# A mixture-of-experts kernel: layer one takes its experts alternately from both ends of their order by count

## The chip, the cores and the metric

One Trainium2 chip, one of its cores. The metric is the device time of the kernel in microseconds, the median of several runs; lower is better. Experts, tiles and sets are counted from 0.

## The reference

Linear attention with 64 heads (8 batches of 8 heads, 576 tokens, 64 features a head) gives 4608 rows of 512. Then two mixture-of-experts layers with 8 experts and one expert per row:

```python
def _moe_ref(x, modality_id, w_gate, modality_bias, w1, w2):
    logits = x @ w_gate + modality_bias[modality_id]
    e_idx = np.argmax(logits, axis=1)
    ...
    for e in range(E):
        mask = e_idx == e
        if not mask.any():
            continue
        h = np.maximum(x[mask] @ w1[e], 0.0)
        out[mask] = gate_w[mask, None] * (h @ w2[e])
```

`w1[e]` is 512 by 1024, `w2[e]` 1024 by 512, all in float32: 4 MB for one expert. Layer two is the same without the modality bias and with a second gate, a sigmoid of `x @ w_output_gate`. How many rows each expert gets follows from the inputs. Worked out from the reference with its inputs, layer one has the counts 1, 0, 29, 0, 0, 5, 2258 and 2315 for experts 0 to 7, so five experts are used; layer two uses all eight (753, 557, 485, 156, 387, 455, 214, 1601).

## The kernel before

**Stages.** About 507 us of attention in 32 steps of two heads, in which the rows of x are stored to `x_tokens` in HBM and each row's token number and weight are scattered into the expert's bin (`bins[0]`). Then layer one in tiles of 128 rows, 43 turns of the tile loop of which 40 hold rows, then layer two likewise (`L` 0 and 1). The rows of a tile are gathered from HBM by the numbers in a bin (`ids`, L466, then `gather`, L473, both on the POOL queue, five tiles ahead); the result of layer one is scattered by token to `y_tokens`, that of layer two to `out` (L495).

**A tile.** On PE, turn `t` of the loop is: first product of tile t (L1272 to L1274, 8 groups of 3 matmuls of 512 columns, two halves); in layer one the transposes of the finished rows of tile t-2 for layer two's router (L1339); transposes of the gathered rows of tile t+1 (L1299); second product of tile t-1 (L1284 to L1286, 8 groups of 3); in layer one the router's logits of tile t-2 (L1367); transposes of tile t's hidden rows (L1379). Products are taken in two parts of float32, a rounded high one and the rest: three matmuls in place of one. ACT makes the high parts (`xh` L657, `hh` L674), DVE the low ones (`xl` L1021, `hl` L1047); ACT's L644 and DVE's L1018 take the two halves of the hidden rows with a relu, DVE's L1041 scales the result into `ys`. In layer one, every fourth tile also takes part in a ranking (`choose2`, `rank2`, `locate2`) that places rows in layer two's bins.

**Weights.** An expert's weights are a set: four pieces of 1 MB, two of `w1` (the W1 half), two of `w2` (the W2 half). `raw` holds one set as loaded. `wts` holds two sets, each in a high and a low part; set g lies in place g % 2. A set is split from `raw` into `wts` by ACT (`round_pieces`, L522: the high part) and DVE (`low_pieces`, L693: the low part). Which tile splits which set stands in the table `turn`, which `plan` writes: the split of set g+1 begins in the tile of set g whose index within its set equals `EARLY`, or in the set's last tile if that comes earlier. In turn t, ACT and DVE do the W1 half, in turn t+1 the W2 half. ACT then issues the load of the set after (`load_after`, L294): its W1 half in turn t+1, its W2 half in turn t+2, each once `raw` is free of the split before. After the last split it loads one more set, which nobody uses. A tile's first product waits for the W1 half of its set (`s_low[L][1]`), its second product for the W2 half.

**The order of experts.** `tables` (L863) gives each expert a key and a rank by it. In layer one: first the expert that had most rows after six of eight batches (`pick_first`; set 0 is loaded and split during the attention, set and rows of tiles 0 to 2 are taken ahead of `tables`), then the used ones by rising count, unused ones last. Every use of the order follows `t_rank` (row numbers `rowi`, tiles per set, `second`, `after`). Layer two goes by falling count, expert 0 first. Layer one's tiles per set are so 19, 1, 1, 1 and 18.

**Loads by SP.** `load_second(L)` loads set 1 once `tables` has written `second[L]` (L893). Behind it on SP's queue: the wait for `plan` (L363), then for i in 0 to 3 the wait until all loads of piece i in layer one have landed and been split (L368), and the load of piece i of layer two's set 0; then the wait for tile 44's rows and `load_second(1)`. At the start of layer two ACT rounds that set in L538 (`round_first`) and DVE makes its low part in L701.

**Queues at the start of layer one.** DVE runs `tables(0)` in turn 0, after tile 0's work, and `plan(0)` in turn 1. ACT waits for `plan` at the start of turn 2. POOL waits for `rowi` (written at the end of `tables`), issues the fetches of row numbers of tiles 3, 4 and 5, then the gather of tile 3, the fetch of 6, the gather of 4.

Of the kernel before, what the change touches and what calls it, by code (L numbers as in the profile page):

```python
# [30 lines left out]
XG = 5  # L31
NXO = 3
NY = 3
EARLY = 2
PICK = 6
SOON = 3
G = 4
# [49 lines left out]
def build(nc, q, k, v, w_phi, modality, w_gate1, bias1, w1a, w2a, w_gate2, w_out2, w1b, w2b, const, out):  # L87
    f32, f32r, i32, bf16 = mybir.dt.float32, mybir.dt.float32r, mybir.dt.int32, mybir.dt.bfloat16
    ALU, ACT, AX = mybir.AluOpType, mybir.ActivationFunctionType, mybir.AxisListType
# [6 lines left out]
    with ctx:  # L96
# [13 lines left out]
        def sem(name):  # L110
# [12 lines left out]
        t_v = sb("t_v", [P, 2, E])  # L123
        t_s = sb("t_s", [P, 2, E])
        t_key, t_rank, t_k, t_end, t_a, t_b, t_d = (sb("t_" + n, [P, E]) for n in
                                                    ("key", "rank", "k", "end", "a", "b", "d"))
        t_m = sb("t_m", [P, 2, E, E])
        t_es, t_last = sb("t_es", [P, E]), sb("t_last", [P, 1])
# [5 lines left out]
        ex, nv, r0, t0 = (sb("j_" + n, [P, TILES]) for n in ("ex", "nv", "r0", "t0"))  # L134
# [163 lines left out]
        def _(eng):  # L298
# [36 lines left out]
            second_reg = [ctx.enter_context(eng.register(f"second{L}")) for L in range(2)]  # L335
            def load_second(L):
                eng.wait_ge(s_sets, L + 1)
                eng.load(second_reg[L], second[L][0:1, 0:1])
                e = eng.snap(second_reg[L])
                for i in range(PPS):  # L340
                    eng.wait_ge(s_low[L][i], 1)
                    raw_load(eng, L, e, i, s_raw[L][i])
# [342 lines left out]
        def _(eng):  # L685
# [20 lines left out]
            def step(ins):  # L706

                nonlocal steps
                steps += 1
                ins.then_inc(s_r, 1)  # L710
                eng.wait_ge(s_r, steps)
# [151 lines left out]
            def tables(L):  # L863
# [18 lines left out]
                else:  # L882
                    step(eng.scalar_tensor_tensor(t_key[:, :], t_v[:, 0, :], float(E), c_("prio"), ALU.mult, ALU.add))
                step(eng.tensor_tensor(t_m[:, 0], t_key[:, :].unsqueeze(1).broadcast_to(ee),
                                       t_key[:, :].unsqueeze(2).broadcast_to(ee), ALU.is_gt))
                step(eng.tensor_reduce(t_rank[:, :], t_m[:, 0], AX.X, ALU.add))
                step(eng.tensor_tensor(t_m[:, 0], t_rank[:, :].unsqueeze(1).broadcast_to(ee),
                                       c_("tile")[:, 0:E].unsqueeze(2).broadcast_to(ee), ALU.is_equal))
                eng.tensor_tensor(t_m[:, 1], t_m[:, 0], t_v[:, 1, :].unsqueeze(1).broadcast_to(ee), ALU.mult)
# [27 lines left out]
            def plan(L):  # L917
# [23 lines left out]
                step(eng.tensor_tensor(r0[:, :], c_("tile"), r0[:, :], ALU.subtract))  # L941
                step(eng.tensor_scalar(t0[:, :], nv[:, :], float(P), None, ALU.is_le))
                step(eng.tensor_scalar(nv[:, :], c_("tile"), t_end[:, E - 1:E], None, ALU.is_lt))
                step(eng.scalar_tensor_tensor(t0[:, :], r0[:, :], float(EARLY), t0[:, :], ALU.is_lt, ALU.mult))
                step(eng.scalar_tensor_tensor(t0[:, :], r0[:, :], float(EARLY), t0[:, :], ALU.is_equal, ALU.add))
                step(eng.tensor_tensor(nv[:, :], nv[:, :], t0[:, :], ALU.mult))
                step(eng.tensor_scalar(t0[:, :], ex[:, :], 1.0, None, ALU.add))
                step(eng.scalar_tensor_tensor(t0[:, :], ex[:, :], t_last[:, :], t0[:, :], ALU.is_lt, ALU.mult))
# [452 lines left out]
```

## Time and profile before

| | |
|---|---|
| median of 3 runs | 1662.55 us (1660.87 to 1669.14) |
| profiled execution | 1657.9 us, span 1656.0 us |
| PE busy | 1555.1 us, 94% of the span |
| DVE, ACT, POOL busy | 823.2, 616.1 and 440.3 us |
| attention | to about 507 us |
| layer one | first matmul at 508.6 us |
| layer two | first rows at 1128.7 us |

The profile's page gives each engine's busy time, its groups of instructions by line with the idle time ahead of them, and the DMA issues. The timeline gives single instructions with start and duration, and in brackets the idle time before one and what ended it. Matmuls are pipelined, so their starts say more than their durations: at the full clock 512 columns start every 0.23 us. A table by windows gives the busy time of each engine in a stretch, the granted clock of TensorE (1.00 is full) and what the DMA engines moved.

### The profile page before, as it was taken

The numbers are of one execution on the slowest core, as the hardware profiler recorded it, in microseconds if no ns is written. First come the engines' busy times: TensorE is split into PE (matmuls) and PEld (weight loads), VectorE is DVE, ScalarE is ACT, GpSimd is POOL, SyncE is SP. The second block draws the span as 40 slices with busy tenths as digits, with TensorE's granted clock in tenths as the row PEclk, the third lists the DMA queues.
The fourth block names the chain that finished last, engine by engine and source line by source line (L and its number), as shares of the span: only waits on it lengthen the run. The fifth ranks groups of instructions, "written<-read, shape, count | busy, mean of one in ns | idle before, by whom it ended". The sixth has DMA issues, their size and how long they took to land. (4 is left out here: it accounts for less than half of the span.)

```text
span 1656.0 us, 32380 instructions
## 1 busy us (share of the span) xinstructions
PE 1555.1 (94%) x9755; PEld 1317.7 (80%) x9755; DVE 823.2 (50%) x1553; ACT 616.1 (37%) x1052; POOL 440.3 (27%) x435
## 2 busy tenths in 40 slices
PE   7999999999998999999599999965999999999996
PEld 5888888888887888888478888854888888888875
DVE  3777777777776433234543323356424223344344
ACT  4666666665651322222422222231322112233332
POOL 2122122123373232233032233224222222222211
PEclk9999999999999999999799999977999999999998
DMA  5333333335624411111462111103414111432343
GB/s 125 85 78 86 80 81 78 81 86 137 174 67 142 147 40 40 40 40 34 159 235 87 40 40 39 40 13 134 153 39 145 48 40 36 150 124 105 105 142 110
DMA packets 184196, 149.94 MB, mean 91 GB/s; under 512 B 131403, under 2 KB 150219, under 8 KB 183504
## 3 DMA queue, kind: packets, MB, share of 16 engines
q1 hardware_dynamic: 143040, 54.92, 12.9%
q0 software_dynamic: 19968, 46.40, 8.8%
q10 hardware_dynamic: 21008, 46.24, 7.8%
q8 instruction: 110, 1.80, 0.5%
q14 instruction: 70, 0.57, 0.1%
HBM read 114.32 MB, written 32.66 MB: 89 GB/s over the span
## 5 line engine op out<-in xcount | busy, mean ns | idle before, releaser
L1272 PE MATMUL bank<-wts,xh 128*128 (+1 forms) x640 | 260.1, 406 | 32.4 <-DVE wts L693 21.5
L1284 PE MATMUL bank<-wts,hh 128*128 (+1 forms) x640 | 257.9, 403 | 3.3 <-DVE hl L1047 3.3
L1274 PE MATMUL bank<-wts,xl 128*128 (+1 forms) x640 | 253.4, 396 | 0.0
L1273 PE MATMUL bank<-wts,xh 128*128 (+1 forms) x640 | 253.3, 396 | 0.0
L1286 PE MATMUL bank<-wts,hl 128*128 (+1 forms) x640 | 251.1, 392 | 0.0
L1285 PE MATMUL bank<-wts,hh 128*128 (+1 forms) x640 | 249.9, 391 | 0.0
L674 ACT ACTIVATE hh<-bank 128x512 fp32r<-128x512 f32 x172 | 93.8, 595 | 372.0 <-PE bank L1379 371.8
L1018 DVE TENSOR_SCALAR hid<-bank 128x512 f32<-128x512 f32 x86 | 59.4, 691 | 262.0 <-PE bank L1274 261.8
L1041 DVE TENSOR_SCALAR ys<-bank,pair 128x512 f32<-128x512 f32 x86 | 64.4, 749 | 237.9 <-PE bank L1286 236.2
L1272 PEld LDWEIGHTS bank<-wts,xh 128*128 128x128 f32 x640 | 122.4, 191 | 58.6 <-issue 34.8
L1233 PE MATMUL p_n<-kvs,qp 128*128 128x100 f32 (+1 forms) x1280 | 160.9, 276 | 3.1 <-ACT kvs L564 1.0
L1233 PEld LDWEIGHTS p_n<-kvs,qp 128*128 128x128 f32 (+1 forms) x1280 | 142.3, 180 | 20.5 <-ACT kvs L564 10.4
L495 POOL DMA_INDIRECT y_tokens<-ys,pair x43 | 43.4, 1010 | 384.3 <-DVE ys L1041 364.4
L1274 PEld LDWEIGHTS bank<-wts,xl 128*128 128x128 f32 x640 | 122.1, 191 | 26.2
L495 POOL DMA_INDIRECT out<-ys,pair x43 | 43.8, 1018 | 371.4 <-DVE ys L1041 371.4
L1284 PEld LDWEIGHTS bank<-wts,hh 128*128 128x128 f32 x640 | 120.7, 189 | 26.8 <-issue 4.2
L1286 PEld LDWEIGHTS bank<-wts,hl 128*128 128x128 f32 x640 | 120.5, 188 | 26.6
L1273 PEld LDWEIGHTS bank<-wts,xh 128*128 128x128 f32 x640 | 122.3, 191 | 24.0 <-issue 0.2
L1285 PEld LDWEIGHTS bank<-wts,hh 128*128 128x128 f32 x640 | 120.8, 189 | 23.2
L1047 DVE TENSOR_TENSOR hl<-bank,hh 128x512 fp32r<-128x512 f32 x172 | 110.9, 685 | 51.7 <-ACT hh L674 51.7
L693 DVE TENSOR_TENSOR wts<-raw,wts 128x2048 f32 x44 | 99.0, 2289 | 62.2 <-ACT wts L522 62.2
L644 ACT ACTIVATE hid<-bank 128x512 f32<-128x512 f32 x86 | 51.5, 598 | 200.0 <-PE bank L1274 191.4
(250 smaller groups left out, 2561.6 us busy)
## 6 DMA issues: line engine op xcount, KB each, us to landing
raw<-in_moe_w ACTq DMA_DIRECT2D x44, 1024.0 KB, 7.4
raw<-in_moe_w SPq DMA_DIRECT2D x16, 1024.0 KB, 8.0
qs<-in_q SPq DMA_DIRECT2D x64, 128.0 KB
ks<-in_k SPq DMA_DIRECT2D x64, 128.0 KB
vs<-in_v SPq DMA_DIRECT2D x64, 128.0 KB
x_tokens<-xo SPq DMA_DIRECT2D x32, 256.0 KB, 2.7
wts<-raw POOLq DMA_DIRECT2D x4, 1024.0 KB, 4.6
bins<-pair,idx POOLq DMA_INDIRECT x83, 3.6
```

Source lines behind the costliest of these rows:

```text
L495: eng.indirect_dma_start(y_dram if L == 0 else out, bass.IndirectOffsetOnAxis(ap=pair2[:, n, 0:1], axis=0), ys[n % NY][:, :], None, bounds ...
L674: eng.activation(hh[:, half * 4:half * 4 + 4, :].rearrange("p a n -> p (a n)"), src[:, :], ACT.Copy).then_inc(s_hh, 1)
L693: eng.tensor_tensor(wts[:, bass.ds(g % 2, 1), 1, cols], raw[:, i, :].unsqueeze(1), wts[:, bass.ds(g % 2, 1), 0, cols].bitcast(f32), ALU.su ...
L1041: eng.tensor_scalar(ys[m % NY][:, :], b_y[:, :], pair2[:, m, 1:2].bitcast(f32), None, ALU.mult).then_inc(s_y, 1)
L1047: eng.tensor_tensor(hl[:, part, :].rearrange("p a n -> p (a n)"), src[:, :], hh[:, part, :].rearrange("p a n -> p (a n)").bitcast(f32), AL ...
L1233: last = eng.matmul(p_n[h][0:m, c * NW:(c + 1) * NW], qp[:, g, cols], kvs[:, h, g, :], start=g == 0, stop=g == 1)
L1272: eng.matmul(dst[:, :], xh[:, c, :], wh, start=c == 0, stop=False)
L1273: eng.matmul(dst[:, :], xh[:, c, :], wl, start=False, stop=False)
L1274: last = eng.matmul(dst[:, :], xl[:, c, :], wh, start=False, stop=c == DC - 1)
L1284: eng.matmul(b_y[:, :], hh[:, c, :], wh, start=c == 0, stop=False)
L1285: eng.matmul(b_y[:, :], hh[:, c, :], wl, start=False, stop=False)
L1286: last = eng.matmul(b_y[:, :], hl[:, c, :], wh, start=False, stop=c == FC - 1)
```

## The change

`EARLY` becomes 3 in layer one and stays 2 in layer two: a set of more than three tiles splits the next one in its tile 3. `load_second(0)` waits for the rows of tiles 3 and 4 as well before it issues set 1. `tables(0)` gets seven DVE instructions that turn a rank r of n used experts into max(min(2r - 1, 2n - 2r), 0), and leave it where that minimum is not above 0 (rank 0 and the unused ones).

```diff
-EARLY = 2
+EARLY = (3, 2)
...
             def load_second(L):
                 eng.wait_ge(s_sets, L + 1)
+                if L == 0:
+                    for t in range(SOON, XG):
+                        eng.wait_ge(s_xin[t], 16)
                 eng.load(second_reg[L], second[L][0:1, 0:1])
...
                 step(eng.tensor_reduce(t_rank[:, :], t_m[:, 0], AX.X, ALU.add))
+                if L == 0:
+                    step(eng.tensor_scalar(t_b[:, :], t_v[:, 0, :], 0.0, 2.0, ALU.is_gt, ALU.mult))
+                    step(eng.tensor_reduce(t_last[:, :], t_b[:, :], AX.X, ALU.add))
+                    eng.tensor_scalar(t_a[:, :], t_rank[:, :], 2.0, -1.0, ALU.mult, ALU.add)
+                    step(eng.tensor_scalar(t_b[:, :], t_rank[:, :], -2.0, t_last[:, :], ALU.mult, ALU.add))
+                    step(eng.tensor_tensor(t_a[:, :], t_a[:, :], t_b[:, :], ALU.min))
+                    step(eng.scalar_tensor_tensor(t_b[:, :], t_a[:, :], 0.0, t_rank[:, :], ALU.is_le, ALU.mult))
+                    step(eng.scalar_tensor_tensor(t_rank[:, :], t_a[:, :], 0.0, t_b[:, :], ALU.max, ALU.add))
...
-                step(eng.scalar_tensor_tensor(t0[:, :], r0[:, :], float(EARLY), t0[:, :], ALU.is_lt, ALU.mult))
-                step(eng.scalar_tensor_tensor(t0[:, :], r0[:, :], float(EARLY), t0[:, :], ALU.is_equal, ALU.add))
+                step(eng.scalar_tensor_tensor(t0[:, :], r0[:, :], float(EARLY[L]), t0[:, :], ALU.is_lt, ALU.mult))
+                step(eng.scalar_tensor_tensor(t0[:, :], r0[:, :], float(EARLY[L]), t0[:, :], ALU.is_equal, ALU.add))
```

`step` lets DVE wait for the instruction's end. `SOON` is 3 and `XG` 5, so the added waits are those for tiles 3 and 4.

## Rows read from the trace of the kernel before

**Rows 1.** The page: busy time by engine, and the costliest group of instructions by line

```profile
PE 1555.1 (94%) x9755; PEld 1317.7 (80%) x9755; DVE 823.2 (50%) x1553; ACT 616.1 (37%) x1052; POOL 440.3 (27%) x435
...
L1272 PE MATMUL bank<-wts,xh 128*128 (+1 forms) x640 | 260.1, 406 | 32.4 <-DVE wts L693 21.5
```

**Rows 2.** Timeline (start, us, engine, line): first matmuls of tiles 24 and 39

```profile
861.76 0.48 PE L1272 MATMUL bank<-wts,xh 128*128 x1
...
1066.58 0.50 PE L1272 MATMUL bank<-wts,xh 128*128 x1
```

**Rows 3.** Timeline of PE: first matmuls of tiles 19, 20, 21 and 22

```profile
764.56 0.48 PE L1272 MATMUL bank<-wts,xh 128*128 x1
...
779.85 0.50 PE L1272 MATMUL bank<-wts,xh 128*128 x1 [1.53 <-DVE wts L693]
...
800.72 0.79 PE L1272 MATMUL bank<-wts,xh 128*128 x1 [7.06 <-DVE wts L693]
...
829.27 0.79 PE L1272 MATMUL bank<-wts,xh 128*128 x1 [12.96 <-DVE wts L693]
```

**Rows 4.** Timeline of ACT and its queue in tile 21, and of DVE in tile 20

```profile
809.82 2.74 ACTq L294 DMA_DIRECT2D raw<-in_moe_w  x4
815.54 1.91 ACT L522 ACTIVATE wts<-raw 128x2048 f32 x1 [5.74 <-DMA raw<-in_moe_w]
...
790.99 8.90 DVE L693 TENSOR_TENSOR wts<-raw,wts 128x2048 f32 x4 [3.12 <-ACT wts L522]
...
800.47 1.27 DVE L1047 TENSOR_TENSOR hl<-bank,hh 128x512 fp32r<-128x512 f32 x2
```

**Rows 5.** Windows: length, busy us of five engines, granted clock, DMA share, GB/s

```profile
535.00:540.00 5.00, 2.49 (x11) 2.06 (x11) 3.61 (x15) 1.66 (x4) 2.95 (x3) 0.83 0.50 145
...
840.00:850.00 10.00, 10.00 (x54) 8.51 (x54) 3.92 (x12) 4.07 (x3) 0.00 (x0) 1.00 0.89 342
...
1600.00:1610.00 10.00, 7.21 (x27) 5.69 (x26) 3.66 (x4) 1.54 (x3) 2.00 (x2) 0.83 0.19 54
```

**Rows 6.** Timeline of several engines, start of layer one, tiles 1 to 4

```profile
517.94 0.17 DVE L879 TENSOR_SCALAR t_a<-t_v 128x8 f32<-128x8 f32 x1
...
520.98 3.27 SPq L294 DMA_DIRECT2D raw<-in_moe_w  x4
...
528.24 0.75 DVE L1041 TENSOR_SCALAR ys<-bank,pair 128x512 f32<-128x512 f32 x1 [2.04 <-PE bank L1286]
...
528.83 0.47 PE L1272 MATMUL bank<-wts,xh 128*128 128x512 f32 x1
...
531.24 0.94 POOL L473 DMA_INDIRECT xin<-x_tokens,pair  x1 [2.47 <-DMA pair<-bins,rowi]
...
537.51 0.66 PE L1299 MATMUL bank<-cst,xin 128*128 128x128 f32 x4 [2.51 <-DMA xin<-x_tokens,pair]
...
538.34 0.60 ACT L644 ACTIVATE hid<-bank 128x512 f32<-128x512 f32 x1 [8.58 <-DVEq L957]
...
546.73 0.48 PE L1272 MATMUL bank<-wts,xh 128*128 x1
...
560.31 0.48 PE L1272 MATMUL bank<-wts,xh 128*128 x1
```

**Rows 7.** DMA issues: median us to landing of row gathers; landings of weight pieces (L294)

```profile
xin<-x_tokens,pair POOLq DMA_INDIRECT x43, 3.5
...
DMA to landing us min/median/max: 4.9/7.5/16.1
```

**Rows 8.** Timeline of PE in layer two: a set's first matmul after an idle

```profile
1603.06 0.64 PE L1272 MATMUL bank<-wts,xh 128*128 x1 [2.79 <-issue]
```

**Rows 9.** Timeline, end of layer one and start of layer two, PE and ACT

```profile
1082.63 0.49 PE L1284 MATMUL bank<-wts,hh 128*128 x1 [1.12 <-DVE hl L1047]
...
1112.94 7.29 ACT L538 ACTIVATE wts<-raw 128x2048 fp32r<-128x2048 f32 x4
...
1128.73 1.11 PE L1299 MATMUL bank<-cst,xin 128*128 128x128 f32 x4 [16.15 <-DMA xin<-y_tokens,pair]
```

## The prediction

> **What bounds the kernel now.** I read the page's engine line first: PE is busy for 94% of the span [rows 1]. So time is to be had only where PE stands idle or runs at its lower clock. Where it waits is in the groups by line: L1272, the first matmul of a tile, waited 21.5 us for DVE's L693, the second step of a weight split [rows 1]. The timeline of PE says where those waits lie. Over tiles 24 to 39 of layer one, which nothing disturbs, a tile takes (1066.58 - 861.76) / 15 = 13.65 us from first matmul to first matmul, the ranking in every fourth tile included [rows 2]. That is the fair price of a tile. Tiles 19 and 24 start at 764.56 and 861.76: 97.20 us for five tiles, whose fair price is 68.25, so **28.95 us are lost** [rows 2, 3].
>
> Why there: PE waits for a split ahead of tiles 20, 21 and 22 [rows 3], so tiles 19, 20 and 21 are a set each. That agrees with the router's counts (2315 rows, then 1, 5 and 29, then 2258). A set's 4 MB are issued only when the set before is split and `raw` is free, and three sets in a row want them within a tile each: at 809.82 four pieces are issued, and ACT gets the first at 815.54, having idled 5.74 us for it [rows 4]. After the two long idles PE works at its lower level (1.2 GHz; the other is 2.4): the first matmul lasts 0.79 us there, after the idle of 1.53 it lasts 0.50 [rows 3].
>
> A second, smaller loss is at the start of layer one. The first matmuls of tiles 2 and 3 are 17.90 us apart [rows 6], 4.25 over the fair price. PE idled 2.51 us for tile 3's rows; that gather was issued at 531.24 and used at 537.51, 6.3 us for what takes 3.5 at the median, and before it POOL had idled 2.47 us for the row numbers [rows 6, 7]. From 520.98 on SP's four pieces of set 1 were in flight [rows 6]. The clock was 0.83 from 535 to 540 [rows 5]; the lower clock after the idle is the rest of the 4.25.
>
> **The new order.** With five used experts the seven new instructions map ranks 1, 2, 3, 4 to 1, 3, 4, 2: the tiles per set become 19, 1, 18, 1, 1 instead of 19, 1, 1, 1, 18. The number of tiles, matmuls, gathers and stores does not change, nor do counts and order of layer two. Splits fall on tiles 3, 19, 23 and 38. Set 2 is loaded from tile 4 on and split at 19, set 3 from tile 20 and split at 23, set 4 from tile 24 and split at 38: the shortest of these has three tiles, 41 us, for four pieces whose landing took at most 16.1 us each [rows 7]. No wait on a load is left in the layer.
>
> **Middle.** Of the five intervals after tile 19 only the first keeps a split within a one-tile set, with its weights long there. It can be read as it stands: 764.56 to 779.85 is 15.29, 1.64 over, at the full clock [rows 3]. In tile 20 DVE has only the second half of set 2 (two pieces) ahead of ys; tile 3 is such a tile today and lost nothing, 546.73 to 560.31 being 13.58 [rows 6]. Gain 28.95 - 1.64 = **27.3 us**. At the other end of the range the idle of 1.53 grows a little and the clock falls. After an idle of 2.79 us in layer two [rows 8] it was 0.83 over 1600 to 1610 [rows 5], 0.17 x 10 = 1.7 us lost: 25.6.
>
> **End of layer one.** Two one-tile sets now lie at its end. Tile 38 to 39 costs again 1.64 us. Then the second half of set 4 is split during tile 39, and tile 39's second product waits for DVE. Measured from the first matmul of a tile, DVE's first two low pieces end at 790.99 + 8.90 / 2 - 779.85 = 15.6 us [rows 3, 4], ys and two hl after them take 800.47 + 1.27 - 799.89 = 1.85 [rows 4], together 17.45, while today that product starts at 1082.63 - 1066.58 = 16.05 [rows 2, 9]. That is 1.4 late, and PE idles about 2.5 us before it (today 1.12). Idles of 2.51 and 2.79 us were followed by the lower clock, one of 1.53 was not [rows 3, 5, 6, 8], so I take the lower clock here too, at the 1.7 us of layer two. No row shows such a tile behind a layer's last split, so both ends: 0 if the idle stays short and the product isn't late; 3.1, and another 1.7 if the clock falls ahead of tile 39 as well. Sum at the end: 1.64 + 1.4 + 1.7 = **4.7 us lost** (1.6 to 6.4).
>
> **Loads at the end.** After the last split ACT loads one more set that nobody uses; SP waits for its landing before it loads set 0 of layer two. Today that comes in tiles 22 and 23, now after tile 39's start T. The unused W1 half is issued a little before ACT's split in that tile, about T+7.5, the W2 half in tile 40's turn of ACT, about T+18.5 (estimates, from the 15.6 and 17.45 above). At 342 GB/s, 3.1 us per MB [rows 5], or at the median landing of 7.5 us [rows 7], SP issues layer two's pieces at about T+15 and T+27, and the last has landed by T+37. They are needed when ACT starts L538: 1112.94 - 1066.58 = 46.4 [rows 2, 9], plus 3.1 for the late end: T+49.5. So 12 us of room and a cost of nothing. What covers them is the routing of the last tiles and `tables` of layer two, through which PE already waits 16.15 us for its first rows [rows 9]; without that cover each us over T+49.5 costs one. Behind these waits SP has queued only set 1 of layer two, which waits for tile 44's rows anyway.
>
> **Start.** The wait in `load_second` moves set 1 from 520.98 to the landing of tile 4's rows. The fetches and gathers of tiles 3 and 4 then have the DMA engines to themselves: the gather takes 3.5 us, and POOL's 2.47 idle goes. The seven added DVE instructions on 8 columns are, at 0.17 each [rows 6], 1.2 us, with what lies between two 1.3. They delay rowi and POOL's fetches by that. Tile 3's gather is issued at 531.24 - 2.47 + 1.3 = 530.1 and lands at 533.6. PE, which idled 2.51 before 537.51, is ready at 535.0: no idle, full clock, gain **4.25**. The 1.3 us don't reach tile 1, since DVE idles 2.04 before ys at 528.24 [rows 6] and `plan` starts after that. Next late would be `plan`, whose end releases ACT at 538.34 [rows 6]; tile 2's hid is then needed by its transposes a good us before tile 3's start at 546.73 - 4.25 = 542.5, so it isn't late. Bounds: gain 4.25 or 0, if the rows still come late, and 1.3 of loss if the added DVE time shows.
>
> **Split one tile later.** Set 1 is issued when tile 4's rows are there, two POOL issues and a gather after 530.1, about 536.5; four pieces at 3.1 us make 549. ACT comes to the split of tile 3 some 8 us after its first matmul, 550.5. So it costs nothing; at tile 2, about 13 us earlier, ACT would have waited for the later load. The set itself isn't used before tile 19.
>
> **A rule against it.** In the rows the gather took 6.3 us beside set 1's load, against 3.5 [rows 6, 7]. The Trainium skill (DMA: Bandwidth & Descriptors, Issuing engines are not separate DMA queues) says that DMAs of all issuing engines run on the same 16 DMA engines and interleave. By that rule the 8 MB moved to the end of the layer slow the stores and fetches of routing there, which is rival 2; the sum takes nothing for it.
>
> **The sum.** -4.25 - 27.31 + 4.74 = **-26.8 us**. The profiled execution (span 1656.0, time 1657.9) would become 1631.1. It lies 4.65 below the median of the runs shown, 1662.55; the difference is level, not work, so the forecast for the median is 1662.55 - 26.8 = **1635.7**. Best end: -4.25 - 27.3 + 1.6 = -30.0, 1632.6. Worst: 0 + 1.3 - 25.6 + 6.4 + 2.8 (one slowed gather) = -15.1, 1647.5. The range begins at 1627, since a median at the profiled execution's level would be 1657.9 - 30.0 = 1627.9.
>
> **Rivals.**
> 1. The start gives nothing: the chain of fetch and gather on POOL, 1.3 us later, makes tile 3 late, not the load. For it: the margin is 1.4 us. Against: 6.3 against 3.5. 1635.7 + 4.25 = 1640.0.
> 2. The moved loads slow the last group's scatter, fetch and gather, three links on PE's path at 6.3 - 3.5 = 2.8 each [rows 6, 7]: 1644.1. Against: those links come last in the wait of 16.15 us before 1128.73 [rows 9], after the last landing at T+37, on today's axis about 1105.
> 3. The clock stays at 2.4 GHz at the end and tile 39's product isn't late: 1632.6.
> 4. The change doesn't do what it says: the three short sets stay together, or `turn` falls on other tiles. The start alone gives 4.25: 1658.3. Against: the map above, worked out for five used experts.
> 5. **Slower:** set 0 of layer two lands late. Its pieces and the unused ones, eight, go one behind another from T+7.5, the last needed by T+55 (ACT rounds one in 1.91 us [rows 4]). It decides from 5.9 us per MB; at the slowest landing, 16.1 each [rows 7], the last lands at T+136: 81 late, 1717. Slower by 0.5% it is from over 10 us per MB. Against: 3.1 us per MB in 840 to 850 [rows 5].
>
> **Chances.** Forecast 0.62 (own range 1631 to 1640), rival 1 0.12, rival 2 0.10, rival 3 0.08, rival 4 0.05, rival 5 0.03. About 0.5%, 8.3 us, is what a measurement of this kernel can tell from no change: below 1654.2 lie the forecast and rivals 1 to 3, 0.92; within, rival 4, 0.05; slower, rival 5, 0.03. The range 1627 to 1648 takes in all but rivals 4 and 5.
>
> **What will show it.** Start: SP's four pieces of set 1 at about 536, no idle of L1299 for xin, tiles 2 and 3 some 13.6 apart. Middle: one idle of 1.5 us ahead of tile 20, none of ACT for a DMA, tiles 19 to 24 in about 70 us. End: an idle of 1.5 before tile 39, one of about 2.5 before its second product, ACT's L538 without a wait for a DMA, PE's wait for the first rows of layer two still about 16 us. The prediction is wrong if a load is waited for anywhere in layer one, or if the stretch from tile 39's start to layer two's first matmul grows by more than 5 us.

## The result and the profile after

| | before | after |
|---|---|---|
| median of the runs | 1661.71 us (4 runs, 1657.37 to 1669.14) | 1636.91 us (4 runs, 1636.19 to 1640.24) |
| ratio, with its 95% interval | | 0.985 (0.9812 to 0.9889) |
| profiled execution: time, span | 1657.9, 1656.0 us | 1636.26, 1634.4 us |
| first matmul of tile 0 | 508.64 | 511.85 |
| tile 2 to 3 | 17.90 | 13.54 |
| tile 19 to 24 | 97.20 | 69.62 |
| tile 38 to 39 | 13.99 | 16.73 |
| tile 39 to the first matmul of layer two | 68.41 | 72.55 |

The change saves 24.8 us between the medians; 26.8 had been forecast, and 1635.7 for the time. The last five lines of the table are start times and intervals of first matmuls (x-times-W1) in the two timelines of PE. Their differences are +3.21, -4.36, -27.58, +2.74 and +4.14 us. With +0.26 us in the interval from tile 36 to 37 they make -21.6 us, the whole difference of the spans, so nothing else moved by more than hundredths. Layer two takes 12.29 us a tile in both kernels, and 15.34 and 13.88 us for the two tiles at its last split.

The page of after, the engine line of PE and the group that answers to L1272 [rows 1] (busy, mean ns of one | idle before them, and what ended most of it):

```profile
PE 1553.4 (95%) x9755; PEld 1317.6 (81%) x9755; DVE 824.0 (50%) x1560; ACT 616.8 (38%) x1052; POOL 439.6 (27%) x435
...
L1283 PE MATMUL bank<-wts,xh 128*128 (+1 forms) x640 | 258.3, 404 | 15.0 <-DVE xl L1032 8.0
```

The 21.5 us of waiting for the weight split are no longer the largest part of that group's idle time. What is largest now is the 8.0 us behind xl.

The start of layer one, timeline of five engines (start, us, engine, line; in brackets the idle time before it and what ended it), answering to [rows 6]:

```profile
529.82 0.98 POOL L469 DMA_INDIRECT pair<-bins,rowi  x1 [7.01 <-DVE rowi L926]
...
533.63 0.95 POOL L476 DMA_INDIRECT xin<-x_tokens,pair  x1 [0.30 <-issue]
...
538.07 0.60 PE L1310 MATMUL bank<-cst,xin 128*128 128x128 f32 x4
...
540.16 2.21 SPq L294 DMA_DIRECT2D raw<-in_moe_w  x4
...
545.60 0.48 PE L1283 MATMUL bank<-wts,xh 128*128 x1
...
553.17 3.72 ACT L525 ACTIVATE wts<-raw 128x2048 f32 x2 [0.27 <-issue]
...
559.18 0.48 PE L1283 MATMUL bank<-wts,xh 128*128 x1
```

POOL's idle of 2.47 us before the gather is 0.30, PE's transposes of tile 3's rows (L1310) have no idle before them (2.51 us in before), and ACT comes to the split in tile 3's turn (L525) without a wait for a DMA. The set's four pieces (SPq) leave after both gathers.

The middle, timelines of PE, ACT and DVE in tile 19, answering to [rows 3, 4]:

```profile
763.42 0.48 PE L1283 MATMUL bank<-wts,xh 128*128 x1
...
771.12 3.72 ACT L525 ACTIVATE wts<-raw 128x2048 f32 x2 [0.42 <-issue]
...
773.42 4.49 DVE L696 TENSOR_TENSOR wts<-raw,wts 128x2048 f32 x2 [2.00 <-ACT wts L525]
...
778.60 0.50 PE L1283 MATMUL bank<-wts,xh 128*128 x1 [1.42 <-DVE wts L696]
```

One wait of 1.42 us is left of the three of 1.53, 7.06 and 12.96, and it is for the split, not for a load. The four intervals after it are 13.58, 13.58, 13.76 and 13.52 us.

The end of layer one, timelines of PE, ACT, DVE and SP's queue, answering to [rows 9]:

```profile
1024.12 0.50 PE L1283 MATMUL bank<-wts,xh 128*128 x1
...
1032.03 3.72 ACT L525 ACTIVATE wts<-raw 128x2048 f32 x2 [0.42 <-issue]
...
1033.75 0.18 DVE L1015 RECIPROCAL pair<-r_sum 128x4 f32<-128x4 f32 x1
1034.92 4.49 DVE L696 TENSOR_TENSOR wts<-raw,wts 128x2048 f32 x2 [0.99 <-ACT wts L525]
...
1040.85 0.50 PE L1283 MATMUL bank<-wts,xh 128*128 x1 [2.71 <-issue]
...
1057.18 3.86 SPq L294 DMA_DIRECT2D raw<-in_moe_w  x2
...
1057.26 1.12 PE L1350 MATMUL bank<-cst,ys 128*128 128x128 f32 x4 [2.60 <-DVE ys L1052]
1059.12 0.79 PE L1295 MATMUL bank<-wts,hh 128*128 x1
...
1091.36 5.49 ACT L541 ACTIVATE wts<-raw 128x2048 fp32r<-128x2048 f32 x3
...
1107.19 1.12 PE L1310 MATMUL bank<-cst,xin 128*128 128x128 f32 x4 [16.22 <-DMA xin<-y_tokens,pair]
```

Here lie both new losses; RECIPROCAL (L1015) is the last instruction of DVE's position step, which stands ahead of the low pieces in this turn. Tile 39 waits 2.71 us, and its second product (L1295) comes 1059.12 - 1040.85 = 18.27 us after its first matmul, against 16.05 before. Layer two's rounding (L541, three of its four pieces in this view) has no wait for a DMA, and PE waits 16.22 us for layer two's first rows, 16.15 before.

The windows of after around it (length, busy us of PE, PEld, DVE, ACT and POOL, granted clock, DMA share, GB/s):

```profile
1040.00:1050.00 10.00, 9.15 (x44) 7.70 (x45) 2.73 (x6) 1.97 (x4) 5.99 (x6) 1.00 0.38 51
1050.00:1060.00 10.00, 7.40 (x39) 6.27 (x39) 7.14 (x8) 6.21 (x7) 0.98 (x1) 0.82 0.79 247
1060.00:1070.00 10.00, 9.51 (x47) 7.71 (x46) 2.63 (x6) 1.92 (x4) 0.98 (x1) 0.84 1.04 384
```

After the idle of 2.71 us the clock stayed at its upper level; after the one of 2.60 us it fell. The moved loads ran at 384 GB/s while PE had its own work.

### The profile page after: what moved, and what is told of

Same layout as the page of the kernel before. It is cut to its first block and busy times, and to the rows that moved or that the text cites. A ratio compares the mean times of both kernels' runs of the same rounds, so it can differ in the third digit from the quotient of the medians.

```text
span 1634.4 us, 32388 instructions
## 1 busy us (share of the span) xinstructions
PE 1553.4 (95%) x9755; PEld 1317.6 (81%) x9755; DVE 824.0 (50%) x1560; ACT 616.8 (38%) x1052; POOL 439.6 (27%) x435
## 5 line engine op out<-in xcount | busy, mean ns | idle before, releaser
L1295 PE MATMUL bank<-wts,hh 128*128 (+1 forms) x640 | 258.1, 403 | 1.8 <-DVE hl L1058 1.8
L1244 PE MATMUL p_n<-kvs,qp 128*128 128x100 f32 (+1 forms) x1280 | 165.1, 281 | 3.1 <-ACT kvs L567 1.0
L1244 PEld LDWEIGHTS p_n<-kvs,qp 128*128 128x128 f32 (+1 forms) x1280 | 146.1, 184 | 20.8 <-ACT kvs L567 10.4
L1295 PEld LDWEIGHTS bank<-wts,hh 128*128 128x128 f32 x640 | 120.8, 189 | 25.0 <-issue 2.5
```

Source lines behind the costliest of these rows:

```text
L1244: last = eng.matmul(p_n[h][0:m, c * NW:(c + 1) * NW], qp[:, g, cols], kvs[:, h, g, :], start=g == 0, stop=g == 1)
L1295: eng.matmul(b_y[:, :], hh[:, c, :], wh, start=c == 0, stop=False)
```

## The experiments

The first four kernels share one set of runs of before (median 1661.84 us), the next four another (1669.45). Each interval below is one between first matmuls in the timeline of PE, as in the table above.

**Part by part: the added wait.** The changed kernel without it:

```diff
-                if L == 0:
-                    for t in range(SOON, XG):
-                        eng.wait_ge(s_xin[t], 16)
```

> The changed kernel without the added wait of SP: set 1 is loaded as soon as tables has written it; new order and split at tile 3 stay. Theory (the load beside the gather makes tile 3 late): SP issues set 1 at about 12 us after layer one's first matmul, POOL idles for the row numbers again, PE idles 2.5 us or more for tile 3's rows, tiles 2 and 3 are 17.9 us apart or up to 1.3 more (13.54 in the changed kernel), and the time is 4.4 to 5.7 us above the changed kernel's 1636.9: 1641 to 1643. Rival (the chain of fetch and gather on POOL, 1.3 us later through the added DVE work, makes it late, not the load): tiles 2 and 3 stay within 15 us and the time at 1637.

Measured: 1638.49 us, ratio 0.9848 (0.9799 to 0.9897); tile 2 to 3 takes 17.89 us. Timeline of SP's queue, POOL and PE, and PE's first matmul of tile 20:

```profile
525.35 0.94 SPq L294 DMA_DIRECT2D raw<-in_moe_w  x2
...
537.22 0.94 POOL L473 DMA_INDIRECT xin<-x_tokens,pair  x1 [4.07 <-DMA pair<-bins,rowi]
...
540.57 0.96 PE L1307 MATMUL bank<-cst,xin 128*128 128x128 f32 x4 [2.49 <-DMA xin<-x_tokens,pair]
...
782.90 0.61 PE L1280 MATMUL bank<-wts,xh 128*128 x1 [1.52 <-DVE wts L693]
```

With set 1 in flight from 525.35 us (two of its four pieces in this view), POOL waits 4.07 us for the row numbers, where it waited 2.47 in before, and PE 2.49 us for the rows, as before (2.51). So the start's 4.35 us come from the wait, given the later split, and rival 1 (the chain on POOL would make tile 3 late anyway) falls. From POOL's first fetch of row numbers to the gather of tile 3 it is 7.56 us here, 5.97 in before and 3.81 in after. The gather itself, issued when the load is nearly done, takes 3.35 us here and not the 6.3 of before: what the load slows is whatever falls beside it. The median, 1638.49, is only 1.6 us over after's, under the expected 1641 to 1643; its four runs lie between 1634.40 and 1644.85, so it doesn't show the 4.35 us, the intervals of the trace do. Tile 20 costs 1.6 us more here: after an idle of 1.52 us PE went on at its lower level (0.61 us for the first matmul, 0.50 in after; the granted clock is 0.52 from 783 to 786 us, 1.00 in after from 778.6 to 782).

**Part by part: the later split.**

```diff
-EARLY = (3, 2)
+EARLY = (2, 2)
```

> The changed kernel with the split of set 1 at tile 2 again; wait and new order stay. Theory (the later load needs the later split): SP issues set 1 at about 540, ACT comes to the split in tile 2 at about 543.5 and idles 3 to 6 us for the first piece, DVE's low pieces end near 554, PE idles for ys or hl in tile 3's turn some 3 us and its clock may fall: 3 to 6 us above the changed kernel, 1640 to 1643. Rival (the tile of delay is of no use): the same time, 1637, and no idle of PE in tile 3's turn.

Measured: 1645.69 us, ratio 0.9898 (0.9861 to 0.9935). Tile 2 to 3 keeps its 13.54 us and tile 3 to 4 takes 18.06, 4.5 more. Timeline of ACT, DVE and PE:

```profile
548.17 1.92 ACT L525 ACTIVATE wts<-raw 128x2048 f32 x1 [2.02 <-DMA raw<-in_moe_w]
551.57 1.92 ACT L525 ACTIVATE wts<-raw 128x2048 f32 x1 [1.49 <-DMA raw<-in_moe_w]
...
553.77 2.29 DVE L696 TENSOR_TENSOR wts<-raw,wts 128x2048 f32 x1 [0.97 <-ACT wts L525]
...
556.78 0.66 PE L1350 MATMUL bank<-cst,ys 128*128 128x128 f32 x4 [2.53 <-DVE ys L1052]
...
566.57 0.48 PE L1283 MATMUL bank<-wts,xh 128*128 x1
```

ACT, one tile early, stands 2.02 and 1.49 us before the pieces, and PE 2.53 us for ys behind DVE's low pieces. The added wait and the later split therefore belong together: either alone gains nothing at the start. The time lies above the expected 1640 to 1643: of the 9.3 us between the spans of this kernel and after, 4.5 are these, 1.6 a lower clock behind the idle of 1.51 us before tile 20 (0.52 from 786 to 789 us), 2.9 a later tile 0, and 0.3 the last stretch of the layer.

**Part by part: the order.** The order of before, with the wait and the later split kept:

```diff
-                if L == 0:
-                    step(eng.tensor_scalar(t_b[:, :], t_v[:, 0, :], 0.0, 2.0, ALU.is_gt, ALU.mult))
...
-                    step(eng.scalar_tensor_tensor(t_rank[:, :], t_a[:, :], 0.0, t_b[:, :], ALU.max, ALU.add))
```

> The changed kernel with the order of before (tiles per set 19, 1, 1, 1, 18); wait and split at tile 3 stay. Theory (the order is worth 27.6 in the middle and costs 6.9 at the end): tiles 19 to 24 take 97 us again, tile 38 to 39 takes 14.0 instead of 16.7 and the stretch from tile 39 to layer two 68.4 instead of 72.6; 27.6 - 2.7 - 4.1 = 20.8 above the changed kernel, 1657.7, 4 us under the kernel before. Rival (the end costs nothing of its own, the 6.9 us there are the clock's chance): 27.6 above, 1664.5, with 72 us in the last stretch.

Measured: 1658.26 us, ratio 0.9978 (0.9959 to 0.9996). Tile 2 to 3 takes 13.53 us, tile 19 to 24 101.10, tile 38 to 39 14.00, tile 39 to layer two 68.41. First matmuls of tiles 20, 21 and 22 in the timeline of PE:

```profile
776.50 0.49 PE L1275 MATMUL bank<-wts,xh 128*128 x1 [1.45 <-DVE wts L696]
...
798.26 0.79 PE L1275 MATMUL bank<-wts,xh 128*128 x1 [7.93 <-DVE wts L696]
...
827.52 0.79 PE L1275 MATMUL bank<-wts,xh 128*128 x1 [13.53 <-DVE wts L696]
```

The three waits are back, and the two losses at the layer's end are gone. The stretch is 3.9 us longer than in before, 1.6 of it in the intervals before tiles 21 and 22 and 2.5 in the interval from tile 23 to 24; no row names the reason. That the time came as expected (1657.7) is in part chance, since the expected 97 us were 4 short. So the middle's gain and the end's losses are both the order's, and the start's is that of the wait with the later split.

**A half-way order.** Tiles per set 19, 1, 1, 18, 1, by exchanging ranks 3 and 4 only:

```diff
-                    eng.tensor_scalar(t_a[:, :], t_rank[:, :], 2.0, -1.0, ALU.mult, ALU.add)
...
+                    eng.tensor_scalar(t_a[:, :], t_rank[:, :], 3.0, None, ALU.is_equal)
+                    step(eng.tensor_scalar(t_b[:, :], t_rank[:, :], 4.0, None, ALU.is_equal))
+                    step(eng.tensor_tensor(t_rank[:, :], t_rank[:, :], t_a[:, :], ALU.add))
+                    step(eng.tensor_tensor(t_rank[:, :], t_rank[:, :], t_b[:, :], ALU.subtract))
```

> The changed kernel with another order by hand: tiles per set 19, 1, 1, 18, 1 (ranks 3 and 4 of the rising order swapped, four DVE instructions in place of seven). Theory (each short set costs by what stands behind it: a split with its weights long there 1.6 us, a load behind a one-tile set 7.2 us and 2.4 in the next tile; a last set of one tile whose split fell 14 tiles earlier costs nothing): 19 to 20 takes 15.2, 20 to 21 about 20.9, 21 to 22 up to 16, the end is that of before (14.0 and 68.4): 9.6 - 6.9 = 2.7 above the changed kernel, 1639.6. Rival (any two one-tile sets side by side cost about a third of the 29 us each, wherever they stand): then the changed kernel's end is as dear as a middle, and both orders are equal within 1 us; second rival, three in a row are no worse than two per set: 19 above.

Measured: 1647.64 us, ratio 0.9897 (0.9857 to 0.9937). The end costs nearly what it cost before (14.00 and 68.76 us, 13.99 and 68.41 then), but tile 19 to 24 takes 87.21 us. Timeline of PE and ACT:

```profile
803.53 0.79 PE L1280 MATMUL bank<-wts,xh 128*128 x1 [7.95 <-DVE wts L696]
...
818.19 1.91 ACT L525 ACTIVATE wts<-raw 128x2048 f32 x1 [5.78 <-DMA raw<-in_moe_w]
822.31 1.92 ACT L525 ACTIVATE wts<-raw 128x2048 f32 x1 [2.20 <-DMA raw<-in_moe_w]
...
830.24 0.22 PE L1220 MATMUL bank<-oh,ranker 128*128 128x40 bf16 x1 [5.82 <-DVE oh L988]
```

My expectation of the time, 1639.6 us, was 8.0 short. I had counted the wait before tile 21 and not the one that follows it: the second halves of the set are issued a turn later, ACT waits 5.78 and 2.20 us for them in tile 22's turn, and DVE's part of the ranking, behind them, holds PE for 5.82 us.

**The changed kernel once more.**

> The changed kernel once more, as the yardstick of this call. My theory: the attention's end depends on the clock that is granted there and not on the change, so tile 0 starts anywhere in 508.5 to 515 us (508.6 and 511.9 so far in the two kernels), and the intervals of the tiles stay: 13.54 us from tile 2 to 3, about 69.6 us from tile 19 to 24 (up to 71.3 where an idle of 1.5 us before tile 20 is followed by the low clock, as it was in one other kernel), 16.7 us from tile 38 to 39, 72.5 to 73 us from tile 39 to the first matmul of layer two. Median 1635 to 1640 us. The rival, that the later tile 0 (by 3.2 us in the first profile) comes from the change: then it stands at 511 us or later here too, with the low clock in 500 to 510 us.

Measured: 1643.43 us, ratio 0.9827 (0.9802 to 0.9852), with before at 1669.45 beside it. The interval from tile 2 to 3 is 13.54 us and from 38 to 39 16.69. But tile 19 to 24 takes 75.38 us, not 69.6 to 71.3, and the last stretch 75.75. Timeline of ACT and PE in tile 19:

```profile
763.37 0.48 PE L1283 MATMUL bank<-wts,xh 128*128 x1
...
772.00 0.60 ACT L656 ACTIVATE yt<-bank 128x512 f32<-128x512 f32 x1 [5.00 <-remote]
...
782.11 0.79 PE L1283 MATMUL bank<-wts,xh 128*128 x1 [4.87 <-DVE wts L696]
```

ACT stood for 5.00 us where it had stood 2.56 in after, for a releaser that the trace names only "remote", although PE's transposes of that turn were issued at 768.93 as in after (768.98). Its split and all behind it came 3.4 us later. Idles of 4.3 to 5.1 us stand at the same line in every fourth turn from tile 7 to tile 35 of this execution, and idles like them in most such turns of the six kernels' traces that are told of below; in before, in after and in the four kernels above there is none. They are the turns in which POOL issues four scatters into layer two's bins (L425, at 767.34 to 771.27 in tile 19's); the same turn of after has the same four without the idle. In turns without a split the idle hardly shows in the intervals (tile 3 to 19 takes 218.09 us, 217.82 in after); in tile 19's it came through to PE. What it is stays open. The median lies above the expected 1635 to 1640, and the first matmul of tile 0 at 511.54, with a granted clock of 0.66 from 500 to 510 us, as the rival of this kernel had it; this is taken up below, under the level.

**The missed term at the end, first half.** Turn 38 has, on DVE ahead of the low pieces, layer two's position step (`locate2`), which a turn four tiles on from the last group has. Eight of its ten instructions go behind the low pieces:

```diff
                         with eng.If(turns[t] != 0):
                             low_pieces(L, turns[t], range(PPS // 2))
+                    if L == 0 and t - 3 in ends:
+                        locate2_rest(ends.index(t - 3))
```

> The changed kernel, with eight of the ten small VectorE instructions of layer two's position step (1.68 us in all, 1032.25 to 1033.93 in turn 38) moved behind the low parts of the split; the two that TensorE's next step waits for stay. The trace puts the 0.99 us before turn 38's low parts down to ScalarE's rounding. My theory: they really stand behind the position step, so that the low parts start 10.1 to 10.2 us into the turn instead of 10.8 (as in turn 19, which has no such step: 10.0), and tile 38 to 39 takes 16.0 to 16.2 us instead of 16.73. The rival (the rounding is what they wait for): the start stays at 10.8 and the interval at 16.73. The total changes by less than can be measured.

Measured: tile 38 to 39 takes 16.15 us. Timeline of PE and DVE:

```profile
1027.67 0.50 PE L1289 MATMUL bank<-wts,xh 128*128 x1
...
1037.89 4.49 DVE L696 TENSOR_TENSOR wts<-raw,wts 128x2048 f32 x2 [1.72 <-ACT wts L525]
...
1043.82 0.50 PE L1289 MATMUL bank<-wts,xh 128*128 x1 [2.13 <-issue]
```

The low pieces start at T+10.22 instead of T+10.80 (T is the first matmul of the tile), and PE's idle shrinks from 2.71 to 2.13 us, by the same 0.58. So they did wait for the position step, though the bracket named ACT's rounding. The time, 1640.09 us in 2 runs, can't tell, as expected.

**The missed term, second half.** TensorE loads the register that says whether a late tile is used (tiles 32 and up) before its waits instead of behind them:

```diff
                     if t < TILES:
+                        if t >= SURE:
+                            eng.load(used_reg[n % 2], used[L][0:1, t:t + 1])
+                            u_now = eng.snap(used_reg[n % 2])
                         eng.wait_ge(s_xl, n + 1)
...
                         else:
-                            eng.load(used_reg[n % 2], used[L][0:1, t:t + 1])
-                            u_now = eng.snap(used_reg[n % 2])
                             with eng.If(u_now != 0):
```

> The changed kernel, with TensorE's register load that says whether a late tile (32 and up) is used at all moved from behind the wait for the low parts to ahead of it. Tile 20's first matmul came 0.69 us after its low parts ended, tile 39's 1.44 us. My theory: the 0.75 us between them is this register load and what hangs on it, which nothing hides once the tile has had to wait; with the load ahead the first matmul of tile 39 comes 0.7 to 1.0 us after the low parts and tile 38 to 39 takes 16.0 to 16.3 us instead of 16.73; the other late tiles' intervals stay at 13.6 to 13.9 us. The rival (the branch itself takes the time, not the load): 1.4 us and 16.73 us stay. The total changes by less than can be measured.

Measured: tile 38 to 39 takes 16.28 us. Timeline of PE and DVE:

```profile
1036.18 0.49 PE L1283 MATMUL bank<-wts,xh 128*128 x1
...
1046.97 4.49 DVE L696 TENSOR_TENSOR wts<-raw,wts 128x2048 f32 x2 [0.99 <-ACT wts L525]
...
1052.46 0.50 PE L1283 MATMUL bank<-wts,xh 128*128 x1 [2.26 <-DVE wts L696]
```

From the end of the low pieces (1046.97 + 4.49 = 1051.46) to the first matmul it is 1.00 us instead of 1.44. In after tile 20, which has no such register, took 778.60 - 773.42 - 4.49 = 0.69. Of the 0.75 between the two, 0.44 is the load; the other 0.31 is put down to the branch, which no run took out. The bracket changes with it: it said "issue" with the load there, and without it the releaser is DVE's split. The time, 1643.17 us in 2 runs, can't tell here either.

**The split first.** Four losses are left behind splits: at tile 20, at tile 39, at tile 39's second product, and at layer two's last split, which before had too. This kernel asks whether all four come from the place of the split in its turn. The block with ACT's loads and rounding and the one with DVE's low pieces go to its beginning, before the relus of the hidden rows (the same lines are gone from behind xh and xl):

```diff
+                    if early <= t - 2 < TILES - 1:
+                        with eng.If(turns[t - 2] != 0):
+                            load_after(L, t - 2, turns[t - 2], W2H)
...
+                        with eng.If(turns[t] != 0):
+                            round_pieces(L, turns[t], W1H)
                     if 0 <= t < TILES:
                         eng.wait_ge(s_ha, n + 1)
                         eng.activation(hid[:, 0:F // 2], b_ha[:, :], ACT.Relu).then_inc(s_ra, 1)
...
+                    if early <= t - 1 < TILES - 1:
+                        with eng.If(turns[t - 1] != 0):
+                            low_pieces(L, turns[t - 1], range(PPS // 2, PPS))
...
+                        with eng.If(turns[t] != 0):
+                            low_pieces(L, turns[t], range(PPS // 2))
                     if 0 <= t < TILES:
                         eng.wait_ge(s_hb, n + 1)
                         eng.tensor_scalar(hid[:, F // 2:F], b_hb[:, :], 0.0, None, ALU.max).then_inc(s_rb, 1)
```

> The split of a newly loaded set (ScalarE's rounding, VectorE's low part) goes to the start of its turn, before the relu of the hidden rows. My theory: the waits of tile 20 (1.6 us), of tile 39 (3.2 us) and of layer two's last set (15.34 + 13.88 against 2 x 12.29, 4.6 us) come only from the place of the split in the turn. 3.7 us of rounding and 4.5 us of low parts then end some 7 us into a turn of 13.6 us: tile 19 to 20 takes 13.5 to 13.8 us instead of 15.18, 38 to 39 takes 13.8 instead of 16.73, tile 39 to layer two about 69 instead of 72.55, and layer two's last split costs nothing; together 12 to 13 us, a median of 1624 us (1621 to 1628). Rival A: the split ahead of the relus holds these and with them the transposes of the hidden rows and the next rows' low part (xl), so the turn with the split grows by 1 to 3 us in its other half: a gain of 4 to 8 us, 1629 to 1633. Rival B: ScalarE now comes to its wait for the DMA a third of a turn earlier, finds the pieces not landed, and stands with the relu behind it: 1637 or more, with a wait for a DMA at the rounding line.

Measured: **1625.26 us, ratio 0.9728 (0.9702 to 0.9754)**, against 1643.43 for the changed kernel in the same runs. Tile 19 to 20 takes 13.52 us, 38 to 39 14.00, 39 to layer two 69.21, and the last two tiles of layer two 12.29 each. Timeline of ACT, DVE and PE in tile 38, and the page's group by line:

```profile
1025.21 3.72 ACT L525 ACTIVATE wts<-raw 128x2048 f32 x2 [0.42 <-issue]
...
1028.58 4.49 DVE L696 TENSOR_TENSOR wts<-raw,wts 128x2048 f32 x2 [0.99 <-issue]
...
1038.08 0.50 PE L1283 MATMUL bank<-wts,xh 128*128 x1
```

```profile
L1283 PE MATMUL bank<-wts,xh 128*128 (+1 forms) x640 | 257.7, 403 | 8.0 <-DVE xl L1040 8.0
```

The low pieces end at 1033.07, 5.0 us before they are needed, instead of 1.44 before a matmul that is already waiting. Of the group's 15.0 us of idle time, 8.0 are left, those behind xl, which this change doesn't touch. Over the stretches from tile 19 to 24, 38 to 39, 39 to layer two and from layer two's first tile to its last, it gains 1.67 + 2.73 + 3.34 + 4.62 = 12.4 us against the profiled execution of after, as expected. Against that of the changed kernel beside it the same stretches give 7.43 + 2.69 + 6.54 + 4.82 = 21.5, and the medians 18.2, more than expected: in that execution the lower clock and ACT's idles stood at just those waits. Neither rival came. A price stands beside it: tiles 3 to 19 and 24 to 38 take 1.1 and 1.4 us more than in the changed kernel beside it (1.3 and 1.8 more than in after). Why is open.

**Is the order still needed?** The same with the order of before. In the first kernel of this kind only ACT's rounding had been moved; DVE's low pieces had stayed behind xl:

> The split at the start of its turn, with the order of before (three one-tile sets in a row) and the rest of the change. The question is whether the new order is still needed once the split is hidden. My theory: the row of one-tile sets is bound by the chain of a half of raw (load, which landed 16.1 us after its issue in before while both halves were under way, then rounding, low part, next load), which moves as a whole with the split; only the part of the waits that was the late split goes. Tile 19 to 20 takes 13.5 us, and tile 19 to 24 takes 85 to 97 us, against 69.6 with the new order; the median is 15 to 27 us above that of the same kernel with the new order, 1640 to 1652 us. The rival, that the waits there were those of the late split too: 69 to 73 us from tile 19 to 24, and the median within 3 us of the new order's. Rival B: ScalarE, standing in its wait for a DMA at the start of the turn, holds the relu and so the second product as well, and the stretch takes more than the 97.2 us of before.

Measured: 1656.66 us beside 1671.06 for before, ratio 0.99 (0.9868 to 0.9932); tile 19 to 24 takes 93.92 us. The time lies above the expected 1640 to 1652, and tile 19 to 20 took 17.25 us instead of 13.5: with ACT's part alone moved, DVE's low pieces start at T+12 behind xl, and that xl waits for ACT, which had one of its "remote" idles there. Both parts moved, and beside it the split first with the new order again:

> As split_first_oldorder, but with VectorE's low parts moved to the start of the turn too; in that kernel only ScalarE's rounding had been moved, VectorE's low parts came behind xl as before, and tile 19 to 24 took 93.9 us. My theory stands: ScalarE waited there for DMAs (5.8, 2.2 and 1.2 us) and for the low parts that free the halves of raw (2.4 and 8.2 us), so of the 93.9 us only the part goes that the late low parts caused. Tile 19 to 24 takes 82 to 92 us, tile 19 to 20 at most 14 us, the median is 12 to 23 us above split_first beside it. The rival (the waits were those of the late split): 69 to 75 us, and within 4 us of split_first.

> The new order with the split at the start of its turn, once more, as the yardstick beside the old order and to see whether its gain holds on another run: 13.5 to 14 us from tile 19 to 20, 68 to 69 us from tile 19 to 24, 13.8 to 14.1 from tile 38 to 39, 12.3 us for each of the last two tiles, and a ratio to before of 0.970 to 0.978. If the gain had been a chance of the clock, it would come out at 0.98 or above.

Measured, beside 1673.27 for before: old order 1645.94 us, ratio 0.984 (0.9806 to 0.9874), tile 19 to 24 85.17 us; new order **1632.01 us, ratio 0.975 (0.9722 to 0.9778)**, tile 19 to 24 67.96 us and 38 to 39 14.00. Timeline of ACT and its queue in the old order:

```profile
797.15 2.70 ACTq L294 DMA_DIRECT2D raw<-in_moe_w  x4
802.69 1.92 ACT L525 ACTIVATE wts<-raw 128x2048 f32 x1 [5.61 <-DMA raw<-in_moe_w]
806.04 1.92 ACT L525 ACTIVATE wts<-raw 128x2048 f32 x1 [1.44 <-DMA raw<-in_moe_w]
```

ACT waits there for loads, wherever the split stands. So in the stretch from tile 19 to 24 the order is worth 27.6 us against before while the split is late (31.5 against the kernel that has all of the change but the order), and still 17.2 (85.17 - 67.96; 13.9 in the medians) once it is early. 10 to 14 us of its gain there were thus the late split's; the part that is left is the one that an earlier split doesn't remove.

## Why the prediction was right

1. **The middle, -27.3: it measured -27.6.** The wait before tile 20 was forecast at 1.64 us over the fair 13.65 and was 1.53 over it. The old order brought the three waits back. No load is waited for. The lower end of the range also proved real: in the kernel without the wait and in the one with the early split the clock fell here after the same 1.5 us of idle, for 1.6 us. It was not low enough, though: in the second execution of the changed kernel the stretch took 75.38 us, 21.8 under the one trace of before and so outside the 25.6 to 27.3, for ACT's idle of 5.00 us, which no row of before has, and the lower clock behind the 4.87 us that PE then waited.
2. **The start, -4.25: it measured -4.36.** All three signs named came: SP's pieces behind the gathers (at 540.16, which is T+28.3 from tile 0; forecast T+27.9), no idle for xin, 13.54 us from tile 2 to 3. The added DVE instructions take from 522.27 to 523.61, 1.34 us for the 1.3 forecast. Rival 1 had its own experiment and fell. The Trainium skill says that DMAs of all issuing engines run on the same DMA engines and interleave (DMA: Bandwidth & Descriptors, Issuing engines are not separate DMA queues). The traces agree at this place: 4.07 us of POOL's waiting for the row numbers with the load beside it, 0.30 without.
3. **The later split, 0: right**, 13.58 us from tile 3 to 4, and 4.5 us dearer when it isn't later.
4. **The loads at the end, 0: right.** ACT's L541 had no wait for a DMA, and PE's wait for layer two's first rows grew by 0.07 us. Rivals 2 and 5 (slowed links, set 0 late) are out by that, and rival 4 (the change doesn't do what it says) by the middle. The rule of rival 2 was true at the start and had no price at the end, because the loads there ran beside the last tiles' work: they moved 361 GB/s from 1070 to 1075 us, 71 from 1075 to 1080 and 1 from 1080 to 1085, so they were done by about T+37, as forecast (T is 1040.85), and POOL issues the last group's scatters, and behind them the fetches and gathers for layer two's first rows, from 1093.66 on.
5. **The end, +4.7: it measured +6.9** (2.74 + 4.14). This is the term of the sum that was mis-sized, in its two halves.
   - Tile 38 to 39 was priced by tile 19 to 20, at 1.64 over the fair price; it was 16.73 - 13.65 = 3.1 over it, at the full clock (2.7 over before's 13.99, which lay 0.3 over the fair price itself). The two tiles are not alike. In turn 38 the position step of tiles 32 to 35 stands ahead of the low pieces, so they start at T+10.80 and not T+10.00: 0.8 us, of which moving eight instructions gave back 0.6. And a late tile's first product stands behind a register load and a branch, which nothing hides once the tile has had to wait: 0.75 us, of which moving the load gave back 0.44. Together 1.55, the whole difference of 16.73 and 15.18; the runs show 1.0 of it, and the rest is argued.
   - Tile 39's second product was forecast 1.4 us late, and the clock at 1.7. DVE was done with hl at T+17.55, where 17.45 had been forecast. But the wait stands before the transposes that precede the product, and these ran at the low clock already (1.12 us for four): 2.2 late. The product itself took 7.48 us instead of 5.57: 1.9 for the clock. Forecast 3.1, measured 4.1. Rival 3, a clock that stays up, did not come here. That it stayed up before tile 39 was the lucky case: after the same idle, 2.70 or 2.71 us, it fell to 0.50 in the three other traces that have it (the kernel without the wait, the one with the early split, and the changed kernel once more). The prediction chose the level by the length of the idle, and these rows don't bear that out.
6. **The level.** Tile 0 starts 3.21 us later in after than in before, in code that the change does not touch. Windows of the end of the attention stage, before and then after:

```profile
500.00:510.00 10.00, 7.99 (x58) 6.97 (x59) 3.96 (x15) 1.13 (x3) 0.00 (x0) 1.00 0.11 31
```

```profile
500.00:510.00 10.00, 9.82 (x44) 8.94 (x44) 1.54 (x8) 0.12 (x1) 0.00 (x0) 0.50 0.01 2
```

   PE worked at its lower level there. Over the profiled executions of all kernels tile 0 starts between 508.51 and 516.93 us, and the kernels with the whole change in them span that range: 508.51 with eight instructions moved and a clock of 1.00 in this window, 511.54 with 0.66 in the changed kernel once more, 516.93 with 0.75 and the register load moved. So the 3.2 us can't be put down to the change, though with one trace of before it isn't shown that before spreads likewise. This also says how near to count the hit: 1636.91 against 1635.7 is closer than that chance allows one to claim, and the spans give 24.8 us of gain for the change itself (21.6 + 3.2), 2.0 under the forecast, which is the mis-sized end (2.2).

## What to carry to other kernels

Price a moved piece of work by the turn it moves into, not by the turn it left: read on every engine what else that turn holds ahead of it, and what an engine does between its wait and its first instruction, since a register load that other work hides can show in full behind a wait (0.44 us here). When an order of the work is tuned around a wait, ask also whether the awaited work could start earlier in its own turn; here that gave another 12 us at the four places, less about 3 in the other turns, with the same instructions. A load that is moved out of the way needs its user moved too, or the wait only changes its place.

## What the runs showed of the hardware that was not expected

- The length of a short idle doesn't tell the clock behind it. After 1.42 us (after) and 1.53 (before) PE went on at its upper level, after 1.52 (the kernel without the wait) and 1.51 (the early split) at its lower one; it stayed up after 2.71 us in one execution and was down after 2.71 in the next of the same kernel (0.50 and 0.79 us for the first matmul of tile 39; granted clock 1.00 and 0.50). A wait thus costs its own length and, in some executions, more: 1.6 us at tile 20. For tile 39 to layer two no such price comes out: it took 72.55 us in after, and 75.75, 72.93 and 72.87 in the three executions in which the clock fell before tile 39 as well.
- ACT's idles with the releaser "remote", 2.4 to 6.6 us in about every fourth turn of layer one, are there in one execution of the changed kernel and not in the other. The median of before rose from 1661.8 to 1669.5 us between the comparisons without them and those with them; whether they are the cause isn't shown, as before has a trace only from the first time.
